# The channel product of a mixing layer: 64 plain float32 matmuls in place of 192 on rounded halves

## The reference

```python
theta = x @ w_theta
zr, zi = x * np.cos(theta), x * np.sin(theta)
y = np.einsum('ts,bsd->btd', w_tok_r, zr) + np.einsum('ts,bsd->btd', w_tok_i, zi)
u = x + y
return u + np.maximum(u @ w_ch, 0.0)
```

## Time and profile before

| | |
|---|---|
| median of 3 runs | 577.35 us (575.19 to 579.12) |
| the profiled execution, span from its first to its last instruction | 573.2 us |
| PE busy | 539.4 us, 94% of the span |
| DVE, ACT, POOL busy | 282.4, 174.7, 233.2 us |
| L1302, the channel product | 192 matmuls, in 480 to 573 us |

### The profile page before, as it was taken

How to read it: one execution, slowest core, us unless ns; L and a number is a source line. 1 busy time by engine, 2 the same in 40 slices (tenths; PEclk the granted TensorE clock), 3 DMA queues, 4 the chain that set the end, 5 groups by cost and what they waited for, 6 DMA issues and landing times.

```text
span 573.2 us, 8964 instructions
## 1 busy us (share of the span) xinstructions
PE 539.4 (94%) x3168; PEld 486.5 (85%) x3168; DVE 282.4 (49%) x614; ACT 174.7 (30%) x431; POOL 233.2 (41%) x183
## 2 busy tenths in 40 slices
PE   1878889889999999999999999999999999999997
PEld 1656667578899998899999888988799999999997
DVE  7999698956754222212222222255666662205033
ACT  3878889422212111111110001153544431001010
POOL 4666667905600550008100230031399788262500
PEclk9999899979999999999999999999999999999999
DMA  6864441222010040001200020000021123332202
GB/s 242 284 216 158 169 142 51 74 77 73 8 67 1 1 146 1 0 0 73 73 0 0 1 82 1 1 0 1 0 56 57 55 83 83 114 107 59 79 15 96
DMA packets 19045, 39.40 MB, mean 69 GB/s; under 512 B 1600, under 2 KB 9792, under 8 KB 19008
## 3 DMA queue, kind: packets, MB, share of 16 engines
q1 hardware_dynamic: 19008, 38.94, 20.7%
HBM read 35.79 MB, written 3.15 MB: 68 GB/s over the span
## 4 chain that ended last, share of the span: by engine, by line
PE 83%; DVE 10%; issue 4%; ACT 2%; DVEq 0%; POOL 0%; DMA 0%; ACTq 0%
PE bank L919 22%; PE bank L935 21%; PE bank L1279 17%; PE bank L1149 6%; PE bank L1302 6%; PE bank L583 3%; PE bank L554 2%; PE bank L569 2%; DVE neg_s L394 1%; DVE probsT L405 1%; PE bank L596 1%; DVE xn L819 1%; PE bank L952 1%; PE bank L1285 1%; ACT probs L520 1%
## 5 line engine op out<-in xcount | busy, mean ns | idle before, releaser
L919 PE MATMUL bank<-xnT,w1h 128*128 128x384 f32 (+1 forms) x512 | 131.8, 338 | 1.7 <-DVE xnT L834 1.7
L919 PEld LDWEIGHTS bank<-xnT,w1h 128*128 128x128 f32 x512 | 93.2, 189 | 3.7 <-issue 1.6
L883 ACT ACTIVATE hTh<-bank 128x384 fp32r<-128x384 f32 x64 | 31.4, 492 | 192.9 <-PE bank L919 192.9
L919 PE MATMUL bank<-xnT,w1l 128*128 128x384 f32 (+1 forms) x256 | 86.2, 337 | 0.0
L842 DVE SCALAR_TENSOR_TENSOR hTl<-bank,hTh 128x384 fp32r<-128x384 f32 x64 | 35.6, 558 | 89.8 <-ACT hTh L883 89.8
L935 PE MATMUL bank<-w2h,hTh 128*128 128x512 f32 x192 | 76.0, 396 | 0.0
L935 PE MATMUL bank<-w2h,hTl 128*128 128x512 f32 x192 | 75.3, 392 | 0.0
L935 PE MATMUL bank<-w2l,hTh 128*128 128x512 f32 x192 | 75.1, 391 | 0.0
L1279 PE MATMUL bank<-ring_h,z_hi 128*128 128x384 f32 x192 | 65.9, 343 | 0.0
L1279 PE MATMUL bank<-ring_h,z_lo 128*128 128x384 f32 x192 | 64.4, 335 | 0.0
L1279 PE MATMUL bank<-ring_l,z_hi 128*128 128x384 f32 x192 | 64.3, 335 | 0.0
(11 more groups left out here) (108 smaller groups left out, 998.9 us busy)
## 6 DMA issues: line engine op xcount, KB each, us to landing
raw<-wtokT SPq DMA_DIRECT2D x24, 384.0 KB, 3.3
raw<-w SPq DMA_DIRECT2D x8, 1024.0 KB, 5.3
k_raw<-kdup SPq DMA_DIRECT2D x16, 424.0 KB, 4.9
v<-vwin SPq DMA_DIRECT2D x8, 704.0 KB, 4.0
q_raw<-qT SPq DMA_DIRECT2D x8, 384.0 KB, 3.4
outT<-out_sb SPq DMA_DIRECT2D x16, 192.0 KB, 1.9
raw<-w_theta SPq DMA_DIRECT2D x1, 1024.0 KB, 5.5
raw<-w_ch SPq DMA_DIRECT2D x1, 1024.0 KB, 5.2
```

The costliest lines, as they stand in the source:

```text
L919: last = nc.tensor.matmul(h_bank[f % 2][:, 0:CN], wt[slot][:, d, fs], tokens(low, d), start=first, stop=(d == DC - 1 and wt is w1l))
```

## The change

`uTh` and `uTl` become one float32 tile `uT`, which ACT copies out of the bank. `channels(n)` multiplies the raw w_ch, as it was loaded, by `uT`, both of type F32: one matmul for each e and d instead of three. The split of w_ch on ACT and DVE goes, and so do `u_low` and the sum on DVE; L1241's successor adds `uT` directly. PE waits for the load of w_ch and for ACT's copies, where it waited for DVE's halves.

```diff
--- before.py
+++ after.py
@@ -979,14 +979,11 @@
         wtl = placed("wtl", 8, [P, DC, DM], F32R)
         x2Th = placed("x2Th", 16, [P, 2, DC, P], F32R)
         x2Tl = placed("x2Tl", 20, [P, 2, DC, P], F32R)
-        uTh = placed("uTh", 0, [P, HALVES, DC, CN], F32R)
-        uTl = placed("uTl", 12, [P, HALVES, DC, CN], F32R)
+        uT = placed("uT", 0, [P, HALVES, DC, CN])
         z_hi = [placed(f"z_hi{b}", kb, [P, TILES, 2, DM], F32R) for b, kb in enumerate((64, 88))]
         z_lo = [placed(f"z_lo{b}", kb, [P, TILES, 2, DM], F32R) for b, kb in enumerate((124, 32))]
         frac = placed("frac", 148, [P, 2, 2, DM])
         trig = placed("trig", 156, [P, 2, 2, DM])
-        wch = placed("wch", 148, [P, DC, DM], F32R)
-        wcl = placed("wcl", 156, [P, DC, DM], F32R)
         ring_h = [placed(f"ring_h{s}", kb, [P, 2, CN], F32R) for s, kb in enumerate((24, 112, 118))]
         ring_l = [placed(f"ring_l{s}", kb + 3, [P, 2, CN], F32R) for s, kb in enumerate((24, 112, 118))]
         out_sb = placed("out_sb", 56, [P, 2, CN])
@@ -999,13 +996,13 @@
 
         theta_loaded, ch_loaded = sem("theta_loaded"), sem("ch_loaded")
         tok_loaded = [sem(f"tok_loaded{s}") for s in range(2)]
-        c_hi, ch_hi, theta_split, ch_split, tok_split = sem("c_hi"), sem("ch_hi"), sem("theta_split"), sem("ch_split"), sem("tok_split")
+        c_hi, theta_split, tok_split = sem("c_hi"), sem("theta_split"), sem("tok_split")
         x2T_mm, x2T_hi, x2T_split = sem("x2T_mm"), sem("x2T_hi"), sem("x2T_split")
         theta_mm, round_step, frac_ready, trig_ready = sem("theta_mm"), sem("round_step"), sem("frac_ready"), sem("trig_ready")
         abs_ready = sem("abs_ready")
         z_ready, z_high, z_split = sem("z_ready"), sem("z_high"), sem("z_split")
-        ring_used, y_mm, u_high, u_split = sem("ring_used"), sem("y_mm"), sem("u_high"), sem("u_split")
-        v_mm, u_summed, out_ready = sem("v_mm"), sem("u_summed"), sem("out_ready")
+        ring_used, y_mm, u_copied = sem("ring_used"), sem("y_mm"), sem("u_copied")
+        v_mm, out_ready = sem("v_mm"), sem("out_ready")
         out_stored = [sem(f"out_stored{s}") for s in range(2)]
 
         MIX = [(b, th) for b in range(BATCH) for th in range(HALVES)]
@@ -1209,48 +1206,29 @@
             for t in range(TILES + 1, TT + 2):
                 rotation_scalar(act, t)
             act.wait_ge(z_split, TT)
-            act.wait_ge(ch_loaded, 16)
-            nc.scalar.activation(wch[:, :, :], raw_ch, ACT.Copy).then_inc(ch_hi, 1)
             for k in range(len(MIX) * DC):
                 th, d = MIX[k // DC][1], k % DC
                 act.wait_ge(y_mm, k + 1)
                 if k >= HALVES * DC:
 
                     act.wait_ge(out_ready, k - HALVES * DC + DC - d)
-                nc.scalar.activation(uTh[:, th, d, :], mix_bank[th][d][:, 0:CN], ACT.Copy).then_inc(u_high, 1)
+                nc.scalar.activation(uT[:, th, d, :], mix_bank[th][d][:, 0:CN], ACT.Copy).then_inc(u_copied, 1)
 
         def mixing_vector(dve):
-            def u_low(n):
-                th = MIX[n][1]
-                for d in range(DC):
-                    dve.wait_ge(u_high, n * DC + d + 1)
-                    nc.vector.tensor_tensor(uTl[:, th, d, :], mix_bank[th][d][:, 0:CN],
-                                            uTh[:, th, d, :].bitcast(F32), ALU.subtract).then_inc(u_split, 1)
-
             def outputs(n):
                 th = MIX[n][1]
-                dve.wait_ge(u_split, (n + 1) * DC)
                 for e in range(DC):
                     k = n * DC + e
                     if k >= 2:
                         dve.wait_ge(out_stored[k % 2], 16 * (k // 2))
-                    nc.vector.tensor_tensor(out_sb[:, k % 2, :], uTh[:, th, e, :].bitcast(F32),
-                                            uTl[:, th, e, :].bitcast(F32), ALU.add).then_inc(u_summed, 1)
-                    dve.wait_ge(u_summed, k + 1)
                     dve.wait_ge(v_mm, k + 1)
                     nc.vector.scalar_tensor_tensor(out_sb[:, k % 2, :], mix_bank[th][e][:, 0:CN], 0.0,
-                                                   out_sb[:, k % 2, :], ALU.max, ALU.add).then_inc(out_ready, 1)
+                                                   uT[:, th, e, :], ALU.max, ALU.add).then_inc(out_ready, 1)
 
             for t in range(TILES + 1, TT + 3):
                 rotation_vector(dve, t)
-            dve.wait_ge(ch_hi, 1)
-            nc.vector.tensor_tensor(wcl[:, :, :], raw_ch, wch[:, :, :].bitcast(F32),
-                                    ALU.subtract).then_inc(ch_split, 1)
             for n in range(len(MIX)):
-                u_low(n)
-                if n >= 1:
-                    outputs(n - 1)
-            outputs(len(MIX) - 1)
+                outputs(n)
 
         def mixing_tensor(pe):
             def mix(n):
@@ -1293,14 +1271,13 @@
 
                 th = MIX[n][1]
                 if n == 0:
-                    pe.wait_ge(ch_split, 1)
-                pe.wait_ge(u_split, (n + 1) * DC)
+                    pe.wait_ge(ch_loaded, 16)
+                pe.wait_ge(u_copied, (n + 1) * DC)
                 for e in range(DC):
                     es = slice(e * P, (e + 1) * P)
                     for d in range(DC):
-                        for m, (wt, ut) in enumerate(((wch, uTh), (wch, uTl), (wcl, uTh))):
-                            last = nc.tensor.matmul(mix_bank[th][e][:, 0:CN], wt[:, d, es], ut[:, th, d, :],
-                                                    start=(d == 0 and m == 0), stop=(d == DC - 1 and m == 2))
+                        last = nc.tensor.matmul(mix_bank[th][e][:, 0:CN], raw_ch[:, d, es], uT[:, th, d, :],
+                                                start=(d == 0), stop=(d == DC - 1))
                     last.then_inc(v_mm, 1)
 
             for n in range(len(MIX)):
```

## The result

| | before | changed |
|---|---|---|
| median, first comparison (3 runs each) | 577.35 us | 584.39 us (583.69 to 584.40) |
| ratio, 95% interval | | 1.0126 (1.0090 to 1.0162) |
| median, second comparison (17 and 5 runs) | 576.44 us | 584.52 us |
| ratio, 95% interval | | 1.0151 (1.0128 to 1.0173) |
| span of the first profile | 573.2 us | 581.9 us |

The changed kernel is slower, by 7.0 us in the first comparison and by 8.1 in the second, and both intervals stay clear of 1; 585.7 (+8.3) was forecast.

What follows compares the result with a forecast made beforehand. PE was taken to bound the kernel, with the channel product wholly on its path; 64 x (0.650 - 0.520) = +8.3 us, all other terms 0, took 577.35 to 585.7 us, with an 8 in 10 range of 580 to 591.

Steps and rivals of the forecast that it cites:

- The product is wholly on the path: Channel product (L1302) in the mixing stage: all its 33.30 us lie on the chain, with DVE and ACT only following.
- Everything removed on DVE and ACT is worth 0: Split of w_ch, 16 subtractions (8.6 us) and 16 sums (11.6 us): removing them gains 0, since PE never idles for them.
- The new waits cost 0: PE's waits for the w_ch load, ACT's four copies and a freed bank: all hidden, cost 0.
- Four sweeps per plain matmul of full width, 0.650 us: Channel product: 64 plain matmuls at 0.650 us replace three rounded ones at 0.520 each, +8.3 us.
- The 4.1 us between span and time: Whole kernel: median time 577.35 lies 4.1 us above the profiled span 573.2; the same 4.1 was added to the forecast span.
- How L583 comes to 0.11 us per matmul: Attention product: with 64 stationary columns both halves of the operand stand side by side, so two sweeps' time is enough.
- rival A: Channel product: a plain matmul's two records overlap at any width, 0.327 us against 0.520; time 565.0; chance 0.13.
- The page's four passes: Channel product: the skill page's four passes for true FP32 give +7.7 us, but 0.213 us for L583 where the trace shows 0.11.
- Rival B: Channel product: partial overlap or three sweeps, 0.48 to 0.58 us per matmul, -2.6 to +3.8 us; chance 0.05.
- Rival C: Channel product: weight loads stand bare between records, up to +25.6 us, time 603; chance 0.04.
- there is no room for that: Channel product: at 128 stationary columns both operand halves cannot stand side by side, so the two records run one after the other.

Runs made afterwards that it cites:

- e9_one_four_slots: e4_one with four slots of out_sb instead of two; 553.82 us against 576.61 for the kernel before, ratio 0.9587.
- e4_one: Changed kernel with one rounded matmul, high halves only, per pair of blocks in place of the plain one; 557.16 us, 19.2 under the kernel before.
- e3_relief: Changed kernel with three rounded matmuls, all of high halves, in place of each plain one; 577.86 us against 576.37 for the kernel before, ratio 1.0005.
- e1_narrow: Changed kernel with each plain matmul of 128 stationary columns cut into two of 64, one half after the other per output block; 592.22 us.
- e7_halves_apart: e1_narrow reordered: all 16 narrow matmuls of the first 64 output columns of the four blocks, then the 16 of the other 64; 619.27 us.
- e2_short: Changed kernel with each plain matmul of 384 moving columns cut into three of 128, stationary operand still 128 wide; 589.5 us.
- e5_bf16_cross: Kernel before with the two products that have a low half on bfloat16 operands, types mixed in order; 576.36 us against 576.44, ratio 1.0001.
- e8_bf16_grouped: e5_bf16_cross with each output block's four rounded matmuls first, then its eight on bfloat16; 575.05 us against 576.61 for the kernel before, ratio 0.9972.

## Why the prediction was right, and where its reasons were not

- *The product is wholly on the path*: right. The mixes kept 21.84 us, PE stayed without idle time, and in e9_one_four_slots every matmul taken away came off the time (in e4_one all but the 3 to 4 us that two slots of output gave back).
- *Everything removed on DVE and ACT is worth 0*: right, by e3_relief (1.0005).
- *The new waits cost 0*: right; DVE alone waits longer.
- *Four sweeps per plain matmul of full width, 0.650 us*: right in its time, 0.645. The term was 64 x (0.650 - 0.520) = +8.3 and is +8.0. The gap is 2.5 ns per record, the low end of the 2 to 13 ns given, about the one that the transposes showed. That the two records are the two halves of the stationary operand, and that the moving one goes through in two halves, is a picture: the runs show two records per matmul and two clocks per column in each.
- *The 4.1 us between span and time*: not a fixed term. It came from a profiled execution on the fast side of the scatter; in the changed kernel the median lies 2.5 us above the first profile's span (584.39 - 581.9). That is why the time of 585.7 was 1.3 high, while the span of 581.5 was 0.4 low.
- *How L583 comes to 0.11 us per matmul*: wrong. It was put down to the two halves of one stationary operand standing side by side at 64 columns, and rival A and its "against" were weighed by that. The starts in e1_narrow and the order of e7_halves_apart show two different matmuls on different halves of the columns instead, each with the time of all its four sweeps. L583 has the two heads of a pair just there, one in each half; its records of the earlier trace rows then read as two rows of starts, one per head, and not as pairs of one matmul. The distance fits as well: the program has four records of one head before the other's, so the other head's first passes three that wait, as many as in e1_narrow and e7_halves_apart. For L583 itself this is the reading that fits the experiments; no run changed L583.
- *The page's four passes*: the prediction said that the Trainium skill's page "FP8 and Floating Point Precision", section "TensorE Precision Notes" (true FP32 takes four passes), does not agree with L583. With the reading above the times do agree: 0.223 us for 128 columns in e2_short and 0.645 for 384 in the changed kernel, the time of four sweeps each and 5 to 10 ns. What passes through the array in that time no trace here shows.
- *Rival A*, 0.327 us per matmul, needed an overlap at full width; there is none. *Rival B*, three sweeps, fell with it. *Rival C*, bare loads: the loads lie beside the records.
- The forecast rested on an exclusion ("there is no room for that" at 128 columns) that was right for the wrong reason, and so far it was luck: it excluded the overlap of halves, where the overlap was one of neighbours. The same rows would have misled if the change had cut its matmuls to 64 columns: by that reading e1_narrow and e7_halves_apart should have been equal, and they are 7.4 us per product apart.

## What to carry to other kernels

On a path that PE bounds, a plain float32 matmul of 128 stationary and 384 moving columns takes the time of four sweeps, and three rounded ones that of three and a bit: the three win, 0.520 to 0.645 us, however much vector work the plain one saves. The count of columns belongs to that rule. Rounded matmuls of 128 columns in the attention stage of the kernel before (L554) start 0.11 us apart, about the time of two sweeps of 53 ns, where one of 384 columns takes little more than one sweep:

```profile
60.92 0.28 PE L554 MATMUL bank<-k_lo,q_hl 128*128 128x128 f32 x1
61.03 0.28 PE L554 MATMUL bank<-k_hi,q_hl 128*128 128x128 f32 x1
61.14 0.28 PE L554 MATMUL bank<-k_lo,q_hl 128*128 128x128 f32 x1
```

Three would be 0.33 us, where a plain one of 128 columns takes 0.223 in e2_short. That is an estimate from two stages of two kernels, and no run sets the two side by side, but it points the other way.

Before a pace is scaled from another line, ask what else ran on PE at that moment: a group whose output takes half of the partitions may be two streams at once, and a row that counts records in a stretch shows the sum of both. And when a product gets short, look at the stores behind it: in e4_one, with two slots, 4 us of the 22 were given back at the end.

## What the runs showed of the hardware

- A plain float32 matmul leaves two records; each takes about two clocks per moving column (0.82 ns, from 0.1117 us at 128 columns and 0.3225 at 384), with 2.5 ns on top of the two sweeps at 384 and 5 at 128.
- Matmuls on different 64 columns of the array overlap if they stand near one another in the program: 10.47 us per product in turn, 12.15 in groups of four matmuls, 19.55 in groups of sixteen. In e1_narrow and e7_halves_apart the other half's first record starts with three records of the half before it still waiting, so records do not always start in the order of the program.
- A rounded matmul of 384 columns is 13 ns over its sweep, one on bfloat16 about 3; each change of type between neighbours adds about 7 ns (e5_bf16_cross and e8_bf16_grouped).
- The attention stage was granted 0.99 of the clock in one profile of the changed kernel and 0.94 in another, and reached the mixing stage 3.9 us later; that is half of the effect of this change.
